# Reading the expert marks at the head of a tile, splitting a scalar chain around a weight split, and two smaller reorderings

## The reference

```
x, state : (8, 8, 512, 64), (8, 8, 32, 64)
a  = softmax(scale * x @ state^T);  xread = a @ state          # 512 rows for each head
a2 = softmax(scale * state @ x^T);  sread = a2 @ x             # 32 rows for each head
t  = concat(xread, sread), heads side by side                  # 4608 tokens of 512
logits = unit(t) @ unit(expert_emb)^T / tau                    # 8 experts
e = argmax(logits);  gate = softmax(logits)[e]
m = gate * (relu(t @ w1[e]) @ w2[e])                           # 512 -> 1024 -> 512
h = relu(m @ w_in);  out = (s * h * h + b) @ w_out             # 512 -> 2048 -> 512
```

## Time and profile before

| | |
|---|---|
| median of three runs | 1391.1 us |
| the profiled execution's own time | 1393.17 us |
| its span, first to last instruction | 1391.1 us |
| TensorE busy | 1345.2 us, 97% |
| VectorE busy | 645.1 us, 46% |
| ScalarE busy | 506.7 us, 36% |
| share of the chain that ended last | TensorE 81%, VectorE 7%, issue 4% |

### The profile page before, as it was taken

The page is one execution under the profiler, slowest core; times in us unless marked ns, Lnnn a source line. Parts: engine busy times, 40 slices in busy tenths (PEclk is TensorE's granted clock), DMA queues, the critical chain, the costliest instruction groups (busy, mean ns, idle before and its releaser), DMA issues.

```text
span 1391.1 us, 23074 instructions
## 1 busy us (share of the span) xinstructions
PE 1345.2 (97%) x6908; PEld 1105.3 (79%) x6909; DVE 645.1 (46%) x1648; ACT 506.7 (36%) x951; POOL 192.6 (14%) x341
## 2 busy tenths in 40 slices
PE   7998899999999999999999999999999999999996
PEld 5776688877788778779888888888888888888884
DVE  5898546666645664757323223232232332322322
ACT  4885335545434643544222222222222222222221
POOL 2236322221222122200001001000010010100101
PEclk9999999999999999999999999999999999999998
DMA  8755313553512451240100001001010010100000
GB/s 252 224 145 193 115 57 103 180 184 108 184 49 68 149 185 49 71 170 9 48 0 31 32 0 62 0 15 47 0 62 0 0 62 0 62 0 0 31 0 31
DMA packets 71938, 103.61 MB, mean 74 GB/s; under 512 B 40424, under 2 KB 41048, under 8 KB 70624
## 3 DMA queue, kind: packets, MB, share of 16 engines
q1 hardware_dynamic: 57824, 72.16, 15.8%
q0 software_dynamic: 8448, 20.40, 4.4%
q10 hardware_dynamic: 5632, 10.60, 2.0%
HBM read 71.81 MB, written 31.34 MB: 74 GB/s over the span
## 4 chain that ended last, share of the span: by engine, by line
PE 81%; DVE 7%; issue 4%; DMA 2%; DVEq 2%; POOL 1%; ACT 1%; ACTq 0%; POOLq 0%; SPq 0%
PE bank_a L1570 26%; PE bank_n L1589 14%; PE bank_tt L1589 12%; PE bank_a L1492 11%; PE bank_n L1525 10%; DMA xg<-x_tok,g_idx 2%; PE bank_tt L1505 1%; PE bank_n L1423 1%; DVEq L363 1%; POOL slot_tab L497 1%; PE bank_tt L1294 1%; PE bank_a L1275 1%; DVE w_in_lo L1044 1%; DVEq L366 1%; PE bank_l L1556 1%
## 5 line engine op out<-in xcount | busy, mean ns | idle before, releaser
L1212 DVE TENSOR_TENSOR sq<-rel 128x512 f32<-128x512 f32 (+1 forms) x144 | 95.4, 663 | 478.4 <-ACT rel L817 478.4
L817 ACT ACTIVATE rel<-bank_a 128x512 f32<-128x512 f32 (+1 forms) x144 | 82.8, 575 | 534.9 <-PE bank_a L1570 534.9
L1570 PE MATMUL bank_a<-y_hi,w_in_hi 128*128 128x512 f32 (+1 forms) x576 | 218.1, 379 | 1.5 <-DVE y_lo L1204 1.4
L1570 PE MATMUL bank_a<-y_hi,w_in_lo 128*128 128x512 f32 (+1 forms) x576 | 217.6, 378 | 0.0
L1570 PE MATMUL bank_a<-y_lo,w_in_hi 128*128 128x512 f32 (+1 forms) x576 | 217.6, 378 | 0.0
L582 POOL DMA_INDIRECT out_rows<-w_raw,out_id x34 | 32.9, 968 | 714.5 <-DVE w_raw L1223 652.1
L1570 PEld LDWEIGHTS bank_a<-y_hi,w_in_hi 128*128 128x128 f32 x576 | 108.4, 188 | 23.0 <-DVE y_lo L1204 1.8
L1570 PEld LDWEIGHTS bank_a<-y_lo,w_in_hi 128*128 128x128 f32 x576 | 108.4, 188 | 20.6 <-issue 0.2
L1570 PEld LDWEIGHTS bank_a<-y_hi,w_in_lo 128*128 128x128 f32 x576 | 108.4, 188 | 19.9
L1525 PE MATMUL bank_n<-w_hi,hid_hi 128*128 128x512 f32 x296 | 115.5, 390 | 1.5 <-DVE hid_lo L1069 1.5
L1525 PE MATMUL bank_n<-w_hi,hid_lo 128*128 128x512 f32 x296 | 115.4, 390 | 0.0
(11 more groups left out here) (237 smaller groups left out, 2136.3 us busy)
## 6 DMA issues: line engine op xcount, KB each, us to landing
w_raw<-in_moe_w SPq DMA_DIRECT2D x16, 2048.0 KB, 10.6
moe_tok<-yg ACTq DMA_DIRECT2D x38, 272.0 KB, 2.1
x_tok<-x_rows SPq DMA_DIRECT2D x8, 1088.0 KB
y_rows<-moe_tok SPq DMA_DIRECT2D x8, 1088.0 KB, 5.3
x_m<-in_x SPq DMA_DIRECT2D x7, 1024.0 KB, 9.4
win_raw<-in_moe_w_in SPq DMA_DIRECT2D x8, 512.0 KB, 10.7
w_raw<-in_moe_w_out SPq DMA_DIRECT2D x1, 4096.0 KB, 16.2
slot_tab<-w_lo SPq DMA_DIRECT2D x2, 1152.0 KB, 6.6
```

The source lines that it names most:

```text
L817: nc.scalar.activation(rel[:, k, 0:cols], ps_g[k][:, 0:cols], ACT.Relu).then_inc(rel_ready, 1)
L1212: nc.vector.tensor_tensor(sq[:, 0:cols], rel[:, k, 0:cols], rel[:, k, 0:cols], ALU.mult).then_inc(sq_ready, 1)
L1570: last = nc.tensor.matmul(ps_g[n % 2][:, 0:cols], w[:, wc], a[:, c, 0:cols], start=(c == 0 and w is w_in_hi and a is y_hi), stop=(c == DC ...
```

## The change

It has five parts.

1. On ScalarE and VectorE the marks of tiles g and g+1 (four reads) are fetched when round g begins, ahead of `x_lo` or `hidden`, instead of two ahead of each branch. ScalarE also reads its row number there, and stores tile g after `next_w2` instead of before.
2. `gate_scale` is cut in two. `gate_norm` (eight chained steps, up to the first Newton round) stays ahead of `next_w2`; `gate_root` (the other two Newton rounds, the norm and the reciprocal) goes behind it.
3. The loops run to `prev = last - 1`, and the last round is written out without the work for `last+1`.
4. The first attention period is reordered: `turn_scores(0)` ahead of the three `st_transpose`, `embed_states` behind `state_read(0)`; on VectorE `evac_st` behind the subtraction; on ScalarE two `x_evac` behind the exponential.
5. TensorE begins with four products of zeros, 128x320 each, into a bank that is overwritten later.

```
+            zeros = lg_all[:].rearrange("p b t e -> p (b t e)")
+            for _ in range(IDLE):                                   # IDLE = 4
+                nc.tensor.matmul(bank_n2[0][:, 0:B * COLS * E], zeros[:, 0:P], zeros, start=True, stop=True)
...
             def tile(g):                                            # VectorE
+                e, changes = experts(g)
+                e_next, changes_next = experts(g + 1)
                 x_lo(g + 2)
                 gate_logits(g + 3)
-                next_w1(g + 1)
+                next_w1(e_next, changes_next)
                 gate_final(g + 1)
                 hidden_lo(g + 1)
-                gate_scale(g + 2)
-                next_w2(g)
-
-            with dve.Fori(2, last) as g:
+                gate_norm(g + 2)
+                dve.sem_inc(norm_turn, 1)
+                next_w2(e, changes, e_next)
+                gate_root(g + 2)
+
+            with dve.Fori(2, prev) as g:
                 tile(g)
+            gate_final(last)
+            hidden_lo(last)
+            e_a, c_a = experts(prev)
+            e_b, _ = experts(last)
+            next_w2(e_a, c_a, e_b)
...
             def tile(g):                                            # ScalarE
+                e, changes = experts(g)
+                e_next, changes_next = experts(g + 1)
+                row = rows_of(act, g)
                 hidden(g + 1)
...
                 hidden_hi(g + 1)
-                store(g)
-                next_w2(g)
+                next_w2(e, changes, e_next)
+                store(g, row)
...
-            with pe.Fori(2, last_g) as g:
+            with pe.Fori(2, prev) as g:
                 tile(g)
+            turn_hidden(prev)
+            up(last_g)
+            down(prev)
             turn_hidden(last_g)
```

More of the change, by code:

```diff
@@ L443, in _ @@
             sp.sem_inc(load_turn, 1)
-            sp.wait_ge(gate_sq, last + 3)
+            sp.wait_ge(gate_sq, last + 2)
             sp.sem_inc(load_turn, 1)
@@ L548, in _ @@
             last = last_tile(pool)
+            prev = tile_ahead_of_last(pool)
             def result_ids(g):
@@ L560, in _ @@
             gather(4)
-            with pool.Fori(2, last) as g:
+            with pool.Fori(2, prev) as g:
                 gather(g + 3)
                 result_ids(g)
+            result_ids(prev)
             result_ids(last)
@@ L679, in _ @@
                 nc.scalar.activation(e1[:], e1[:], ACT.Exp, scale=-1.0).then_inc(e1_done, 1)
+                if i == 0:
+                    for j in range(2):
+                        x_evac(1, j)
                 if i + 1 < B:
@@ L709, in next_w1, with next_w2 @@
                         nc.scalar.activation(w1_hi[:, c], w_raw[:, c], ACT.Copy).then_inc(w1_hi_done, 1)
-            def next_w2(g):
-                e = expert_of(act, g)
-                with act.If(changes_after(act, g) > 0):
+            def next_w2(e, changes, e_next):
+                with act.If(changes > 0):
                     act.wait_ge(w2_loaded, 16 * e + 32)
@@ L787, in tile @@
                 hidden_hi(g + 1)
-                store(g)
-                next_w2(g)
-            with act.Fori(2, last) as g:
+                next_w2(e, changes, e_next)
+                store(g, row)
+            with act.Fori(2, prev) as g:
                 tile(g)
+            hidden(last)
+            gate_soft(last)
+            result(prev)
+            hidden_hi(last)
+            e_a, c_a = experts(prev)
+            e_b, _ = experts(last)
+            next_w2(e_a, c_a, e_b)
+            store(prev)
             def wout_hi(n):
@@ L1007, in _ @@
                     .then_inc(sh_done, 1)
+                if i == 0:
+                    for k in range(1, B // 2):
+                        evac_st(k)
                 dve.wait_ge(e2_done, 2 * i + 2)
@@ L1045, in win_lo, with experts, next_w1 @@
                     .then_inc(win_ready, 1)
-            def next_w1(g):
-                e = expert_of(dve, g)
-                with dve.If(changes_after(dve, g) > 0):
+            def experts(g):
+                return expert_of(dve, g), changes_after(dve, g)
+            def next_w1(e, changes):
+                with dve.If(changes > 0):
                     for k in range(WS):
@@ L1088, in gate_scale @@
                 assert n_gate[0] == GATE_STEPS - 1
+            def gate_scale(g):
+                gate_norm(g)
+                gate_root(g)
             def gate_final(g):
@@ L1176, in _ @@
             win_lo(0)
-            next_w2(1)
+            e_a, c_a = experts(1)
+            e_b, _ = experts(2)
+            next_w2(e_a, c_a, e_b)
             gate_final(2)
@@ L1438, in _ @@
                     scores(i)
+                if i >= 1:
+                    turn_a1(i - 1)
+                    turn_rows(i - 1)
+                turn_scores(i)
                 if i == 0:
@@ L1442, in _ @@
                         st_transpose(k)
[L1443 to L1446, removed]
                 turn_e2(i)
-                if i == 0:
-                    embed_states()
-                else:
+                if i >= 1:
                     row_logits(i - 1)
@@ L1455, in _ @@
                 state_read(i)
+                if i == 0:
+                    embed_states()
                 if i + 1 < B:
```

76 lines of the change are left out of this document (50 added, 26 removed).

## The result

The changed kernel takes 1412.99 us (median of four, 1410.53 to 1414.66) against 1391.46 us of the kernel before: 1.0154 times as long, 95% interval 1.0134 to 1.0174. The profiled execution took 1414.66 us and spans 1412.6, which is 21.5 us more than before.

A forecast was written before the change was run, and what follows sets the result against it. TensorE, busy 97% of the span, was taken to bound the kernel. Terms 15.0 + 14.0 + 1.9 - 2.2 + 0 = +28.7 us on 1391.1 gave 1419.8 us, range 1398 to 1429.

The forecast's parts named there:

- The splits earlier: Expert rounds with a change: splits of `w_lo` begin 3.1 us earlier, so the 0.90 us wait in `down` goes.
- `xg_lo` later: Expert rounds with a change: root chain and four reads delay `xg_lo`; 2.1 us more a change, +15.0 us for seven.
- The rival in which the reads hide: Expert rounds: the sequencer reads on while the chain runs, `xg_lo` comes early enough, 1375.5 us in all; chance 0.12.
- The clock: Behind TensorE's 3.4 us waits in changes: granted clock falls to half, 2.0 us a change, +14.0 us (0 to 24).
- Loop entry: Start of the expert loop: added reads make `turn_x` 1.3 us late and `up` 0.64: +1.9 us (0 to 2.5).
- Loop exit: End of the expert loop: dropped work lets `y_lo` move ahead by about 2 us: -2.2 us (-2.4 to -1).
- First period: First attention period: reordering and zeros give 0 (-2.5 to +1.6); rival that zeros raise the clock early, 1417.3 us, chance 0.08.

The follow-up runs named there:

- the exchange of the two: Changed kernel with the second half of the root chain moved behind VectorE's four reads, at the head of the next round: ratio 0.9897 to the kernel before.
- The kernel with the waits of 1.75 us: Changed kernel with two of VectorE's four reads moved behind `xg_lo` and the gate logits: ratio 1.0043 to the kernel before.
- the reads put behind: Changed kernel with VectorE's four mark reads moved behind `xg_lo` and the gate logits: ratio 0.9937 to the kernel before.
- both behind: Changed kernel with VectorE's four reads and then the second half of the root chain moved behind `xg_lo` and the gate logits: ratio 1.0123 to the kernel before.

## Why the prediction was right

**The splits earlier.** Right: they begin 3.05 us earlier against `up` (3.59 behind it, 6.64 before), forecast 3.1, and `down`'s 0.90 is gone.

**`xg_lo` later.** Right in mechanism. Splits and `w_in_lo` took 5.69 us (5.68 forecast), the root 1.64 (1.69). From reciprocal to `xg_lo` it was 3.33 us where I had 3.55: the two added reads cost 1.22 and not 1.44. `turn_x` was 1.9 us later than before, not 2.1, and a round with a change took 2.0 us more: 13.75 us in place of 15.0, and 0.5 in rounds ahead of changes that I had at nothing. But the reason I gave for reads that can't hide was only half of it. That a read began 0.10 us after the reciprocal tells of reads behind a chain; behind plain splits they do hide. The rival in which the reads hide had 0.12 from me, and the mechanism it names is real; what decides is the order of chain and reads, as the exchange of the two shows. Even so it promised too much: with the reads hidden 0.5 us a change was left, until TensorE's own read was moved too.

**The clock.** Right, and shown by the run that kept TensorE busy: seven falls of seven, 11.5 us for my 14.0. A fall cost 1.04 to 2.45 us: the granted clock was at half for 3.4 us behind five of the changes and for 6.8 behind two, and the latter cost most. The 2.0 a change was my choice between 0 and 3.4; that the mean of 1.6 lies so near it is in part luck.

**Loop entry.** Right in direction, too large: 1.01 us for 1.9. `turn_x` started 0.27 us behind its ideal place, not 1.3; part of the reads hid, as the lower bound had it. With the reads behind `xg_lo` the entry took 12.22 us again.

**Loop exit.** Right: -2.42 us for -2.2. `y_lo` starts ahead of the last `down`'s end, and the first `dense_up` follows without a wait; the line answers to the earlier trace rows:

```profile
641.23 0.28 PE L1637 MATMUL bank_a<-y_hi,w_in_hi 128*128 128x256 f32 x1
```

**First period.** Wrong: I had 0, with zeros that change nothing because turns were slow at 16.29 in spite of steady work. The fast clock came at 4.9 us in the changed kernel (4.3 to 6.9 in the twelve profiles with zeros), and at 12.8 and 17.8 in the two without. The Trainium skill ("TensorE: Matmul & The Clock Gate", Part 1) says that activity releases the throttle; the trace agrees, and I should have given that rule more than 0.08. Reordering and zeros put TensorE up to 3.3 us ahead at `state_read(1)`; in the changed kernel's profile 1.35 us of that were left.

**Ahead of the loop.** The changed kernel was 2.84 us ahead at the third `up`, a term that I didn't have. About 1.35 us are the first period's. The rest goes with falls that went elsewhere: one at 121 us which the kernel before hadn't, and none at 154, where TensorE waited 1.00 us for gathered rows and not 2.22. Other profiles have falls at 114 to 129, at 151 to 157, at both, or at neither. I count this part, about 1.5 us, as chance and not as the change's; without it the profile would have grown by some 23 us.

So 28.7 us forecast and 21.5 measured: 1.25 less for `xg_lo`, 2.5 for the clock, 0.9 for the entry, 2.8 ahead of the loop and 0.2 at the exit, against 0.5 more in other rounds.

## What to carry to other kernels

Ask of every register read what the sequencer does just ahead of it. In this kernel it was free behind long plain instructions, and behind a chain of steps that wait for each other it cost its full length, so reads go ahead of chains and not behind them. Before a chain is moved behind a block of work, list what waits for what follows the block (here a 0.7 us subtraction that frees a bank). A stall of TensorE can have a second price in the clock: here about 1.6 us for a stall of 3 us, and behind stalls of 1.4 to 2.0 us the clock fell 7 times of 14. Useless products in the stall save it, but taking the stall away saves both.

## What the runs showed of the hardware

- The fall behind a short idle time isn't sure: none of seven behind 0.4 to 0.7 us, five of seven behind 1.75 in one kernel and two of seven behind 1.4 to 2.0 in another, 13 of 14 behind 3.0 to 3.2 (two profiles). The kernel with the waits of 1.75 us also has the largest spread of times (8.9 us over ten executions, against 4.9 over 21 of the kernel before on that chip).
- One wait alone doesn't tell of a fall. In the changed kernel the clock fell at 121.0 us, where no wait just before was longer than 1.15 us, but several shorter ones stood close together.
- Four reads of SBUF into registers (2.9 us) ran wholly under four subtractions of 128x1024 (4.63 us) in the runs with the root chain ahead of the splits.
- The profiles on the chip of four of the experiments (the reads put behind, the first run with the root ahead, both behind, TensorE kept at work) reach the first `up` of the experts at 131.6 to 133.7 us, those on the others at 121.5 to 124.9; the kernel before took 1400.1 us there against 1391.2 to 1391.5. Why isn't known, since I have no profile of the kernel before from that chip; the ratios are taken within a chip.
